# Three mixers behind local attention: token-weight remainders move from GpSimd to VectorE, with sums, x2 and tiles in another order

## The reference, cut to what matters

```python
def _moe_ref(x, w_tok1, w_tok2, w_ch1, w_ch2):            # x: 2 x 768 x 512
    xt = x.transpose(0, 2, 1)
    h = np.maximum(xt @ w_tok1, 0.0) @ w_tok2             # tokens, hidden 256
    u = x + h.transpose(0, 2, 1)
    h2 = np.maximum(u @ w_ch1, 0.0) @ w_ch2               # channels, hidden 1536
    return (u + h2).astype(np.float32)

def _moe2_ref(x, w_theta, w_tok_r, w_tok_i, w_ch):
    theta = x @ w_theta
    cos_t, sin_t = (np.cos(theta), np.sin(theta))
    zr, zi = x * cos_t, x * sin_t
    y = np.einsum('ts,bsd->btd', w_tok_r, zr) + np.einsum('ts,bsd->btd', w_tok_i, zi)
    u = x + y
    return (u + np.maximum(u @ w_ch, 0.0)).astype(np.float32)
```

## Time and profile before

| | us |
|---|---|
| median of three runs | 516.38 (515.48 to 516.88) |
| the profiled execution | 516.6 |
| its span in the trace | 514.8 |
| PE busy | 492.7 |
| PEld busy | 446.4 |
| DVE busy | 329.5 |
| POOL busy | 267.0 |
| ACT busy | 191.7 |

### The profile page before, as it was taken

One profiled execution on the slowest core, in us unless ns is written; L12 is line 12 of the kernel. 1 busy time (PEld: TensorE's weight loads), 2 busy tenths in 40 slices (PEclk: granted clock), 3 DMA queues, 4 the chain that ended last, 5 costly groups with the idle time before them and its releaser, 6 DMA issues.

```text
span 514.8 us, 8394 instructions
## 1 busy us (share of the span) xinstructions
PE 492.7 (96%) x2917; PEld 446.4 (87%) x2917; DVE 329.5 (64%) x797; ACT 191.7 (37%) x413; POOL 267.0 (52%) x315
## 2 busy tenths in 40 slices
PE   7999999998999999987999999979979999999997
PEld 5999999887999999786899989858868899888897
DVE  7998998576433353597523446798885684665452
ACT  6999999453111131144111114232321230331130
POOL 3575566599498884199578882564640130000040
PEclk9999999999999999999999999979989999999999
DMA  7896775422232331104123242132101221000002
GB/s 235 313 320 224 238 225 123 129 81 83 60 85 83 95 104 68 42 19 144 42 73 113 69 129 71 62 122 88 57 1 29 68 87 64 0 1 0 2 31 93
DMA packets 27084, 49.81 MB, mean 97 GB/s; under 512 B 3361, under 2 KB 17697, under 8 KB 27041
## 3 DMA queue, kind: packets, MB, share of 16 engines
q1 hardware_dynamic: 27040, 49.26, 30.1%
HBM read 39.81 MB, written 3.15 MB: 83 GB/s over the span
## 4 chain that ended last, share of the span: by engine, by line
PE 81%; DVE 13%; ACT 3%; issue 2%; DMA 1%; DVEq 0%; ACTq 0%
PE bank L323 59%; PE bank L1753 7%; PE bank L1481 5%; PE bank L1511 4%; PE bank L1514 3%; PE bank L1495 2%; PE bank L1493 2%; DVE bank L1308 1%; DVE split L1279 1%; DVE wsplit L1302 1%; ACT wsplit L916 1%; DVE bank L1297 1%; DVE act_raw L1205 1%; DVE act_raw L1211 1%; DVE zc L1227 1%
## 5 line engine op out<-in xcount | busy, mean ns | idle before, releaser
L323 PE MATMUL bank<-wsplit 128*128 128x512 f32 (+2 forms) x816 | 148.9, 338 | 0.2
L323 PEld LDWEIGHTS bank<-wsplit 128*128 128x128 f32 x816 | 134.4, 188 | 14.2 <-issue 0.8
L710 POOL TENSOR_TENSOR wsplit<-wraw,wsplit 128x512 fp32r<-128x512 f32 (+1 forms) x77 | 101.4, 1317 | 35.6 <-ACT wsplit L883 30.0
L323 PE MATMUL bank<-wsplit,zs 128*128 128x512 f32 (+1 forms) x576 | 103.3, 338 | 0.0
L323 PEld LDWEIGHTS bank<-wsplit,zs 128*128 128x128 f32 x576 | 89.8, 188 | 14.2
L778 POOL TENSOR_TENSOR split<-act_raw,split 128x384 fp32r<-128x384 f32 x12 | 12.5, 1073 | 109.3 <-ACT split L997 109.3
L323 PE MATMUL bank<-split,wsplit 128*128 128x384 f32 x276 | 55.1, 341 | 7.0 <-DVE wsplit L1325 5.6
L652 POOL TENSOR_TENSOR wsplit<-qk_raw,wsplit 64x256 fp32r<-64x256 f32 x46 | 38.0, 825 | 33.6 <-DVE wsplit L1040 33.2
L323 PEld LDWEIGHTS bank<-split,wsplit 128*128 128x128 f32 x276 | 46.8, 188 | 9.7 <-POOL wsplit L710 3.7
L704 POOL CAST wsplit<-wraw 128x512 fp32r<-128x512 f32 (+1 forms) x59 | 35.8, 606 | 36.8 <-PE bank L323 27.5
L323 PE MATMUL bank<-wsplit,tile 128*128 128x512 f32 x144 | 39.7, 429 | 6.9 <-DVE tile L1189 3.8
(11 more groups left out here) (126 smaller groups left out, 751.8 us busy)
## 6 DMA issues: line engine op xcount, KB each, us to landing
wraw<-weights SPq DMA_DIRECT2D x28, 512.0 KB, 3.3
qk_raw<-qk SPq DMA_DIRECT2D x23, 528.0 KB, 4.5
wraw<-weights SPq DMA_DIRECT2D x8, 768.0 KB, 4.0
vt<-v SPq DMA_DIRECT2D x10, 520.0 KB, 4.6
xT<-turned SPq DMA_DIRECT2D x64, 48.0 KB, 2.0
out<-act_raw SPq DMA_DIRECT2D x16, 192.0 KB, 1.9
xT<-turned_early SPq DMA_DIRECT2D x16, 96.0 KB, 2.3
xT<-wraw SPq DMA_DIRECT2D x32, 48.0 KB, 2.0
```

The source lines that it names most:

```text
L323: mm = pe.matmul(dst, lhs(a), rhs(c), start=first and i == 0, stop=last and i == 2, skip_group_check=True)
L710: ins = pool.tensor_tensor(dst[:, cols], src[:, cols], hi[:, cols].bitcast(F32), ALU.subtract)
```

## The change

Four edits, all in the order or the place of work; the arithmetic stays.

1. Sums: `find_sum(0)` and `(1)` leave the u loop and come ahead of the first L1325; each regular product's L1325 is no longer behind a pair of sums of its own round, with the last two sums (6, 7) behind the fourth L1325. ScalarE's `sum_to_hi` pair follows the r1 rounding in place of preceding it.
2. x2 of batch 0: `finish_x2(0, 2)` comes behind the first L1267 (`h1_lo`); GpSimd starts the chunk n = 7 when all of x2 of batch 0 is done (`x2_done` 8), no longer when the tile of the token block is (`tile_lo` 12).
3. Angle tiles: tiles 2 and 3 of x2 are made earlier; in the loop the tile is made before z, on ScalarE ahead of `sines`.
4. The six TOKRI chunks are subtracted by VectorE, one instruction of 1536 columns each (`tokri_to_lo`); GpSimd skips them, and takes each CHAN chunk only when `w_ready` has counted all chunks before it.

```diff
@@ GpSimd
+                if TOKRI <= chunk < CHAN:
+                    continue
                 pool.wait_ge(w_in[i % 2], 16 * (i // 2 + 1))
...
                         if n == PAIR_F + 1:
-                            pool.wait_ge(tile_lo, 2 * T)
+                            pool.wait_ge(x2_done, NC * KD)
...
+                    if chunk >= CHAN:
                         slot = CHAN_AT[chunk - CHAN]
+                        pool.wait_ge(w_ready, i)
...
-                    if TOKRI <= chunk < CHAN:
-                        pool.wait_ge(w_hi, chunk - TOKRI + 1)
-                    else:
-                        round_in_pieces(w_at(slot, 0, 0, width), raw)
+                    round_in_pieces(w_at(slot, 0, 0, width), raw)
@@ ScalarE
-                    if i == 5:
-                        sum_to_hi(0)
-                        sum_to_hi(1)
                 for i, (f, c) in enumerate(REGULAR):
-                    if 1 <= i:
-                        sum_to_hi(2 * i)
-                        sum_to_hi(2 * i + 1)
                     act.wait_ge(r1_ready, b * PRODUCTS + i + 1)
                     act.activation(r1_at(b * PAIR_F, f, 0, c * SC, SC), bank[6 + i % 2][:, 0:SC],
                                    ACT.Relu).then_inc(r1_hi, 1)
+                    sum_to_hi(2 * i)
+                    sum_to_hi(2 * i + 1)
...
+                    if last:
+                        tile_to_hi(B * T + 2)
...
+                    if 1 <= g < B * T - 2:
+                        tile_to_hi(B * T + g + 2)
                     if g >= 2:
                         sines(g)
                         z_to_hi(g, 0)
                     if g:
                         z_to_hi(g, 1)
-                    if g + 2 < B * T:
-                        tile_to_hi(B * T + g + 2)
-                    if g + 3 < len(TOKRI_AT):
-                        round_tokri(g + 3)
+                    if 1 <= g < len(TOKRI_AT) - 2:
+                        round_tokri(g + 2)
@@ VectorE
+            def tokri_to_lo(n):
+                i = TOKRI_IN + n
+                dve.wait_ge(w_hi, n + 1)
+                dve.wait_ge(w_ready, i)
+                dve.tensor_tensor(w_at(TOKRI_AT[n], 1, 0, CHUNK), wraw[:, i % 2],
+                                  w_at(TOKRI_AT[n], 0, 0, CHUNK).bitcast(F32), ALU.subtract).then_inc(w_ready, 1)
...
-                    for i in range(3):
-                        finish_x2(b - 1, i)
+                    finish_x2(b - 1, 0)
+                    finish_x2(b - 1, 1)
...
+                    if b and j == 0:
+                        finish_x2(b - 1, 2)
...
-                        find_sum(0)
-                        find_sum(1)
-                    if i == 6:
-                        sum_to_lo(0)
...
-                    if 1 <= i:
+                    if i < 3:
                         find_sum(2 * i)
                         find_sum(2 * i + 1)
...  (wait for r1_hi, then L1325)
-                    if i == 0:
-                        sum_to_lo(1)
-                    else:
+                    if i < 2:
                         sum_to_lo(2 * i)
                         sum_to_lo(2 * i + 1)
+                    elif i == 2:
+                        sum_to_lo(4)
+                    else:
+                        sum_to_lo(5)
+                        find_sum(6)
+                        find_sum(7)
+                        sum_to_lo(6)
+                        sum_to_lo(7)
...
+                    if last:
+                        tile_to_lo(B * T + 2)
+                        tokri_to_lo(0)
             z_to_lo(0, 1)
             find_angles(1)
...
-            tile_to_lo(B * T + 2)
+            tokri_to_lo(1)
             z_to_lo(1, 0)
+            tile_to_lo(B * T + 3)
             for i in range(2 * KD):
                 finish_x2(B - 1, i)
...  (loop over g)
                         find_angles(g)
                         multiply_x(g)
+                    if g >= 2 and g + 2 < B * T:
+                        tile_to_lo(B * T + g + 2)
+                    if g >= 2 and not (b and s == 0):
                         z_to_lo(g, 0)
                     if g and not (b and s == 0):
                         z_to_lo(g, 1)
-                    if g and g + 2 < B * T:
-                        tile_to_lo(B * T + g + 2)
+                    if 1 <= g < len(TOKRI_AT) - 1:
+                        tokri_to_lo(g + 1)
                     if b == 0 and s >= T - 2:
                         dve.wait_ge(w_ready, len(ORDER))
```

More of the change, by code:

```diff
@@ L757, in _ @@
                     slot = 1 if chunk == TOK2 else chunk - THETA
-                    if TOKRI <= chunk < CHAN:
-                        slot = TOKRI_AT[chunk - TOKRI]
-                    elif chunk >= CHAN:
+                    if chunk >= CHAN:
                         slot = CHAN_AT[chunk - CHAN]
+                        pool.wait_ge(w_ready, i)
                         pool.wait_ge(h2_done, B * BLOCKS)
```

## The result

| | before | changed |
|---|---|---|
| median, us | 516.58 (514.24 to 517.78, 10 runs) | 517.93 (517.12 to 520.43, 10 runs) |
| ratio | | 1.0031 (95%: 1.0017 to 1.0045) |
| profiled execution, us | 516.6 | 517.27 |
| its span | 514.8 | 515.5 |

The time lies in the range given (512.6 to 518.3), but on the other side of no change from where it was forecast (515.2). What is certain in both is that the forecast gain did not come.

A forecast was written before the change was run, and what follows sets the result against it. TensorE was taken as the bound, busy 492.7 of 514.8 us, leaving idle and low-clock time to win. Execution 516.6 - 4.05 (sums, x2, chunk n = 8) + 2.65 (second mixer) = 515.2 us; range 512.6 to 518.3.

The forecast's parts named there:

- The mechanism that it put first: Forecast as summed, 47%: shorter TensorE stalls, then a gap of about 8 us and low clock at mix(5); 514.0 to 516.6.
- what chunk n = 8 takes back: Batch 1, product(2, 0): TensorE waits 0.6 to 0.7 us for GpSimd's later chunk; bounds 0 to 1.5.
- how much later mix(5) starts: Second mixer: mix(5) starts at 402.55 us against 401.9 before, 0.65 us later.
- the slow clock behind it: Mix(5), after TensorE's long idle time: low clock costs 2.0 us, bounds 1.0 and 3.0.
- the clock in small waits: Rival, 16%: the clock also falls in the 1.9 us wait ahead of angles(3), costing 2.0 us; 517.9 us in all.
- Sums: First mixer, regular products: product(1, 1) starts 1.55 us earlier in each batch, with a 1.0 us wait at block(0, 0, 0).
- x2 and sums in batch 1: Batch 1, first mixer: 1.6 us from x2 of batch 0 plus 1.55 us from the sums.
- a sign of being wrong: One of the listed signs: product(2, 0) of batch 1 waits for GpSimd by more than 1.5 us.
- Second mixer up to mix(3): Mix(3) starts at 377.6 against 384.83 us, seven us won, despite waits of 1.9, then 0.7 to 0.8 each round.
- The long wait: Ahead of mix(5): TensorE idles 7.9 us while VectorE waits for all 36 chunks and GpSimd splits two CHAN chunks.
- The doubt about 9.95 us: GpSimd's two CHAN chunks took 9.95 us beside a busy VectorE before; taken as it is, 1.95 us worse.
- the clock falls at the new small wait too: Rival, 16%: low clock also at the 1.9 us wait ahead of angles(3), costing 2.0 us; 517.9 us in all.

The follow-up runs named there:

- number 5: Changed kernel, two runs: first, both Theta chunks one pair later, 525.58 us; second, GpSimd's wait ahead of chunk n = 7 back at tile_lo 12, 518.00 us.
- number 2: Changed kernel plus 36 idle products of 512 columns into PSUM bank 7 between mix(4) and mix(5): 515.88 us, ratio to before 0.9979.
- number 4: Changed kernel with the sums and x2 edits undone, leaving angle tiles and VectorE's token-weight subtraction: 520.82 us, ratio to before 1.0068.
- number 3: Kernel before with only the sums and x2 edits, including GpSimd's later start: 514.30 us, ratio to before 0.9943.
- number 6: Two runs: changed kernel plus 36 idle products ahead of mix(5) and 8 ahead of angles(3), 515.06 us; then the changed kernel itself again, 517.19 us.
- number 1: Changed kernel with VectorE's wait for all 36 chunks and its six turnings moved behind z_to_lo(5, 1): 509.59 us, ratio to before 0.9859.

## Why the prediction was wrong, step by step

The mechanism that it put first is the one that the chip showed, wait for wait; the signs of the parts were right, and their sum fell on the wrong side. The step that failed is the sizes of three terms of the loss: what chunk n = 8 takes back (forecast 0.65 us, measured 1.85, the largest miss), how much later mix(5) starts (0.65, measured 1.5) and the slow clock behind it (2.0, measured 2.2). They were small by some 2.2 us together. A fourth, the clock in small waits, was given to a rival and not to the forecast.

- **Sums.** Forecast 1.55 us a batch with a new wait ahead of the opening block. product(1, 1) of batch 0 came at 123.38 against 125.03, 1.65 us. Right.
- **x2 and sums in batch 1.** Forecast 3.15; product(1, 1) came at 240.22 against 245.21 in the trace before, 4.99, of which 1.65 are batch 0's: 3.34. Right. But number 5 shows that GpSimd's later start, on which most of the 1.6 us for x2 rest, wins nothing once its price is on the bill.
- **Chunk n = 8: the first mis-sized term.** "It waits 0.6 to 0.7": product(2, 0) came at 255.90 against 259.04, so 1.85 of the 4.99 were lost. The wait itself was 1.68 us, over the 1.5 that the prediction had named as a sign of being wrong. The walk added GpSimd's instructions and nothing between them. The trace has 0.66 us more for a transfer that starts only when the first Theta chunk has left its buffer. The rest is a later start (221.89, which is 223.54 with batch 0's 1.65 added, not 223.3) and some stretched instructions (two L704 in 1.50 us, elsewhere 1.29), by the look of it those that ran beside VectorE; no run isolates that. Timeline of GpSimd in the changed kernel:

```profile
241.72 2.67 POOL L710 TENSOR_TENSOR wsplit<-wraw,wsplit 128x512 fp32r<-128x512 f32 x2
245.05 0.74 POOL L721 TENSOR_TENSOR mix_raw<-wraw 128x256 f32<-128x256 f32 x1 [0.66 <-DMA wraw<-weights]
...
249.45 1.50 POOL L704 CAST wsplit<-mix_raw 128x512 fp32r<-128x512 f32 x2
```

- **Second mixer up to mix(3).** With the shift of 3.00 us (angles(1)'s successor at 325.79 against 328.79 in the trace before) taken off: mix(0) at 340.0, forecast 340.15; angles(3) at 350.5, forecast 350.65, with a wait of 1.85, forecast 1.9; the next waits 0.77 each, forecast 0.7 to 0.8; mix(3) at 377.95, forecast 377.6. Right, and the subtraction took 1.75 us, which the sum had at 1.72. The formula in the Trainium skill (VectorE: DVE Perf Modes, The TRN2 errata) gives 1.76, an estimate, since the page has measured it at 512 and 2048 columns: the trace agrees. The terms listed for the cycle add up to 9.2 us, not the 9.3 written; in the trace it is 9.4 from the start of mix(1) to the start of angles(4) (350.37 to 359.78). Two such rounds are where mix(3)'s 0.35 comes from.
- **The long wait: the second term.** Forecast 7.9 us and mix(5) at 402.55; measured 8.3 and 403.3, against 401.8 before. "Two chunks of 3.97 and their hops make 8.0" was 8.3: the two chunks took 4.03 us (382.60 to 386.63) and 4.01 (386.75 to 390.76), with 0.13 and 0.12 of hops ahead of them. That is 0.3; with 0.35 carried over from the cycle (mix(3) came at 377.95, not 377.6) and 0.1 of small differences it makes the 0.75 between 402.55 and 403.3. The 0.1 between 401.9 and 401.8 makes it 1.5 later than before and not 0.65. The doubt about 9.95 us is settled: no stretching with VectorE standing still.
- **The clock behind it: the third.** Forecast 2.0, measured 2.1 by number 2 and 2.2 against the kernel before (10.66 us to angles(6) against 8.48). The mean of the two losses in the earlier trace rows was a guess that came near; the bounds 1.0 and 3.0 say how open it was.
- **The clock in small waits.** The rival "the clock falls at the new small wait too" had 16%. It was weighed as all or nothing for one place, by a full-speed row behind a wait of 1.03 us. It is true in some executions (number 4), and so is a fall at the wait for chunk n = 8, which no rival had. Five of the ten executions of the changed kernel stand at a mean clock of 0.984 to 0.987 and at 518.2 to 520.4 us, the other five at 0.989 or 0.990 and at 517.1 to 517.7; the median lies 0.7 us above the profiled execution by that.

In sum, for the profiled execution: 4.99 won, 1.85 lost on n = 8 and 0.14 more before angles(2), 1.5 and 2.2 in the second mixer, 0.7 slower; forecast 4.05 won, 2.65 lost, 1.4 faster. Of the 2.1 between, the chunk is 1.2, the start of mix(5) 0.85, the clock behind it 0.2 and the 0.14 the rest, and 0.3 more was won than forecast. With the medians, another 0.7. No single term turns the sign: with the chunk at its true 1.85, the sum would still have been 0.2 us faster than before, and the middle of its own range (0.75) would have changed almost nothing. It took the chunk and the long wait together: where a gain of 4.05 and a loss of 2.65 nearly cancel, errors of about 1 us decide the sign.

## What to carry to other kernels

Work taken from one engine drags along what is counted behind it: list every semaphore that the moved step raises, and who waits for its last count. Here one count (all 36 chunks) tied 8 us of another engine's work to the last subtraction. With the subtractions in VectorE's idle places the same kernel was 1.2% faster than before and no longer 0.3% slower; with the wait for that count behind z as well 2.5%, and with two chunks in another order 3%. Before an idle engine's start or order is moved, look where it would wait anyway: in this kernel work ahead of such a wait was free, and behind it cost 7.9 us. And a wait of TensorE as long as the 1.8 to 2.4 us here is to be priced with a slow clock behind it in some of the executions.

## What the runs showed of the hardware

- TensorE's clock fell from 2.4 to 1.2 GHz behind waits of 1.85 us (number 4), 2.35 us (number 3) and 2.36 us (number 6), and not behind waits of the same 1.85 and of 1.68 (changed kernel) and of 2.07 (number 1). Behind 8.3 us it was low in every profile but the filled ones. In three profiles it also fell near 11 us, with only waits of up to 1.3 us since 6 us, so the length of one wait does not tell the whole. Price: 1.4 us (number 6, 2.36 us of wait), 1.5 (number 4), 2.2 (8.3 us) and 2.4 (near 11 us, second run of number 5). The Trainium skill (TensorE: Matmul & The Clock Gate, Part 1) says that the window in which the gate counts activity runs freely against the program, so that one kernel differs from run to run. The profiles agree that it differs; the window itself no run here shows.
- 36 matmuls that nobody reads, put into an idle stretch of 8.3 us, brought the 48 behind it from 10.66 to 8.54 us and the program 2.1 us down.
- Beside GpSimd, VectorE's operations with two SBUF inputs took up to 1.67 us and not 0.69, and GpSimd's own pairs of subtractions 2.99 and not 2.65 (number 1).
